# Unread products between two halves of a layer, a column copy shared by two engines, an earlier weight load, and low parts moved from GpSimd to VectorE

## The chip, the cores and the metric

The kernel runs on one core of one Trainium2 chip. The metric is the device time of one execution, in microseconds. The core has TensorE (PE, matrix products), VectorE (DVE), ScalarE (ACT), GpSimd (POOL) and SyncE (SP, which here only issues DMAs). SBUF is the on-chip memory in which operands lie, PSUM the one into which PE writes.

## What is computed

```python
# attention with hash buckets: 16 heads of 768 x 64
mask = q_bucket[:, :, :, None] == k_bucket[:, :, None, :]
scores = np.where(mask, scale * np.matmul(q, k.transpose(0, 1, 3, 2)), -1e9)
attn = exp(scores - max) / sum
x = (attn @ v), rearranged to (1536, 512)
# first mixture: each token goes to one of 8 experts
logits = x @ w_gate; expert_idx = argmax(logits, axis=1)
for e in range(8):
    xe = x[expert_idx == e]
    out[mask] = gate_w[mask, None] * (np.maximum(xe @ w1[e], 0.0) @ w2[e])   # 512 -> 1024 -> 512
# last layer, all 1536 tokens: 512 -> 1536 -> 512
xn = x / rms * rms_g
return silu(xn @ w_gate) * (xn @ w_val) @ w_out
```

All inputs and the output are float32.

## The kernel before

A float32 operand is held as two bf16 parts: the high part is read in place (the upper two bytes of each word, `upper[...]`), the low part is the difference, written by one subtraction. A product of two float32 matrices is three bf16 products: high by high, high by low, low by high.

**Attention** (to about 233 us) runs head by head, `h` from 0 to 15. PE makes scores (`score_tile`, `score_t_block`), ACT exponentiates them (L1076), and POOL writes the low parts of the probabilities tile by tile (`low_part(h, t)`, L1653) for t = 0, 1, 2, 4, 5; DVE does t = 3 (L1386). PE weighs the values of head h - 1 during head h; its first such product waits for all low parts of that head (`plo_ready`, before L685). The last head's values are weighed after all scores, tile by tile (L769 to L781).

**The first low part.** Ring slot 0 holds the first expert's first matrix (512 x 1024; per partition 4 row blocks `j` of 1024 columns). The low part of its left half is written in four pieces of 128 x 512, one for each j (`first_split`, L1687, semaphore `first_parts`), by POOL between its tiles: j = 0 and 1 after `value_low(15)` of head 14, ahead of `low_part(14, 4)`; j = 2 between `low_part(14, 4)` and `low_part(14, 5)`; j = 3 in head 15 behind `low_part(15, 2)`.

**Routing** (233 to 257 us): DVE works out each token's expert and place in a sorted order (L1404 to L1494), writes `one_hot` rows with which PE gathers the columns of unit 0 (L810) into `window[0]`, and POOL scatters all 1536 rows in sorted order to DRAM (12 indirect DMAs, L1728). From there three transposing DMAs (L586, issued by SP) bring the sorted columns back as `xT`, 8 planes (4 high, 4 low) of 1536 columns, 512 columns for each DMA.

**The mixture** runs ten units: eight experts and two spare ones. For unit u, `hidden(u, f)` (f = 0 to 7; L845, L846, L847) makes the first layer and `outputs(u)` (c = 0 to 3; L865 to L867) the second. PE's order: hidden(0), outputs(0), hidden(1), hidden(2), outputs(1), hidden(3), outputs(2), and so on. Each weight matrix is an item k in a ring of four slots. `split_half(k, side)` on POOL (L1675) writes the low part of half an item (128 x 2048) and raises `w_split`; POOL does these one behind the other from the end of its scatter: (0, 1), (1, 0), (1, 1), (2, 0), (2, 1), ... `hidden(u, 4)` waits for the second half of its item, `hidden(u, 0)` for the first, `outputs` for its item's halves at c = 0 and c = 2. Item 0 is hidden(0), 1 outputs(0), 2 hidden(1), 3 hidden(2), 4 outputs(1).

After each `hidden(u, f)` ACT writes the high part of the activations (L1104) and DVE the low part (L1500, `h_lo`); `outputs(u)` waits for all eight. For units u >= 1 the columns must be copied out of `xT` at a start known only at run time into `window[u % 2]`: `stage(u, planes)` on ACT (L1038), as planes 0 to 6 in one copy and plane 7 in a second, the latter raising `staged`, for which `hidden(u, 0)` waits. For unit 1 it waits for the first two transposes (`columns_in[0]`, `[1]`). Behind it in ACT's order stand the outputs of unit 0 (`take_output_block(0)`), then the activations of unit 1; unit 2's columns are staged in three pieces between those. DVE's order is: activations of unit 0, outputs of unit 0 (L1509, low parts of y), activations of unit 1.

**SP's order** there: the three transposes, a wait for `table_ready`, two register loads of the spare experts' numbers, then the loads of items 4, 5, ... , each behind `slot_free(k)`, which waits until PE has done with item k - 4 (L498 is `load_output`, L493 `load_hidden`).

**The last layer** (from about 410 us) is bound by PE and is not touched.

Of the kernel before, what the change touches and what calls it, by code (L numbers as in the profile page):

```python
# [25 lines left out]
NH = BATCH * HEADS  # L26
# [28 lines left out]
START_AT = 5  # L55
SPLIT_AT = [2, 5]
OUT_AHEAD = 2

# [110 lines left out]
def build(nc, qk, v, proj, w_router, w1, w2, w_gate, w_val, w_out, rms_g, consts, out):  # L171
# [14 lines left out]
    with ctx:  # L186
# [231 lines left out]
        wo_loaded = sem("wo_loaded")  # L418
        wo_split = sem("wo_split")
        staged = [sem(f"staged_{x}") for x in ("even", "odd")]  # L420
        h_ready = sem("h_ready")
        h_hi = sem("h_hi")
        h_lo = sem("h_lo")
# [32 lines left out]
        def _(sp):  # L456
# [127 lines left out]
            for c in range(ROUNDS):  # L584
                tokens = slice(c * GROUP, (c + 1) * GROUP)
                sp.dma_start_transpose(xT_parts.rearrange("p a j c -> p (a j) c")[:, :, tokens], parts[tokens, 0:2 * DM])\  # L586
                    .then_inc(columns_in[c], 16)
            sp.wait_ge(table_ready, 1)
            spare = [sp.value_load(table[0:1, T_EXPERT + n:T_EXPERT + n + 1], min_val=0, max_val=E - 1)
                     for n in range(OVER)]  # L590
            for k in range(RING, 2 * BLOCKS):
                slot_free(k)
                for u in range(BLOCKS):
                    if u >= E and k in (item_of_hidden(u), item_of_output(u)):
                        load_over(u, k, spare[u - E])
                    elif k == item_of_hidden(u):
                        load_hidden(u, u)
                    elif k == item_of_output(u):
                        load_output(u, u)
# [15 lines left out]
        def _(pe):  # L615
# [208 lines left out]
            def hidden(u, f):  # L824
                k, m = item_of_hidden(u), KF * u + f
                if f == 0:
                    if u:
                        pe.wait_ge(staged[u % 2], (u + 1) // 2)
                    else:
                        pe.wait_ge(first_columns, 2 * KD)  # L830
                if u == 0 and f == 0:
                    pe.wait_ge(first_parts, KD)
                elif f % (KF // 2) == 0:
                    pe.wait_ge(w_split, 2 * k + f // (KF // 2))
                if m >= 4:

                    pe.wait_ge(h_lo, m - 3)
                width = widths[u if u < E else u + OVER]
                o = bank(m % 4).shape_from_register(width)
                for j in range(KD):  # L840
                    c = j * F + f * P
                    w_hi, w_lo = upper[k % RING][:, c:c + P, 1], low[k % RING][:, c:c + P]
                    x_hi, x_lo = (window[u % 2][:, a, j, :] for a in range(2))
                    xh, xl = x_hi.shape_from_register(width), x_lo.shape_from_register(width)
                    mm(o, w_hi, xh, start=(j == 0), stop=False)  # L845
                    mm(o, w_hi, xl, start=False, stop=False)  # L846
                    last = mm(o, w_lo, xh, start=False, stop=(j == KD - 1))  # L847
                last.then_inc(h_ready, 1)
# [18 lines left out]
                        last = mm(o, w_lo, hh, start=False, stop=(f == KF - 1))  # L867
                    last.then_inc(y_ready, 1)

            for f in range(KF):  # L870
                hidden(0, f)
            for u in range(EARLY_WIDTHS, E):
                take_width(u)
# [162 lines left out]
        def _(act):  # L1036
# [74 lines left out]
            def stage(u, planes):  # L1111

                lo, hi = planes.start, planes.stop
                if lo == 0:
                    for c in range(2 if u == 1 else ROUNDS):
                        act.wait_ge(columns_in[c], 16)
                    if u > 1:
                        act.wait_ge(h_ready, KF * (u - 1))
                rows = xT[:, bass.ds(starts[u], 2 * KD * NTOK - NTOK + WMAX)]
                part = 2 * KD - 1  # L1120
                to = window[u % 2][:, :, :, :].rearrange("p a j c -> p (a j) c")
                last = copy(to[:, lo:min(hi, part), :],
                            rows[:, lo * NTOK:min(hi, part) * NTOK].rearrange("p (m c) -> p m c", c=NTOK)[:, :, 0:WMAX])
                if hi > part:
                    last = copy(to[:, part, :], rows[:, part * NTOK:part * NTOK + WMAX])
                    last.then_inc(staged[u % 2], 1)
# [19 lines left out]
                    act.wait_ge(table_ready, 1)  # L1146
                    take_start(1)
            act.wait_ge(scattered, 16 * TT)
            stage(1, slice(0, 2 * KD))
            take_output_block(0)  # L1150
            take_start(2)
            for f in range(KF):
# [101 lines left out]
        def _(dve):  # L1254
# [86 lines left out]
            def normalize(h):  # L1341
# [7 lines left out]
                if h >= 2:  # L1349
# [3 lines left out]
                V.tensor_tensor(x_head[h % 2][:, :, :], o[:, :, 0:D], scale.broadcast_to([P, T, D]), ALU.mult)\  # L1353
                    .then_inc(u_free, 1)

            def sum_logits(b):

                own.link(V.reduce_sum(L[:, b * T:(b + 1) * T, :].rearrange("p t e -> p (t e)"),
                                      logit_parts[:, b * T:(b + 1) * T, :, :].rearrange("p t e h -> p (t e) h"), AX.X))
# [12 lines left out]
            for h in range(NH):  # L1372
                if h >= 2:
                    normalize(h - 2)
                if h + 1 < NH:
                    for t in range(T):
                        reduce_tile(h + 1, t)
                        if t == 1 and h % 2 == 0 and h // 2 + 1 < PAIRS:
                            take_blend(h // 2 + 1)
                    maxima(h + 1)  # L1380
                if h == HEADS + 1:
                    dve.wait_ge(u_free, HEADS)
                    sum_logits(0)
                value_sum_rows(h)
                dve.wait_ge(exp_done, UNITS * h + 2 * DVE_TILE + 2)
                V.tensor_tensor(probs_lo[h % 2][:, DVE_TILE, :], probs[h % 2][:, DVE_TILE, :],  # L1386
                                probs_up[h % 2][:, DVE_TILE, :], ALU.subtract).then_inc(plo_dve_ready, 1)
                p = h // 2 + 2
                if h == hash_slot(p) and p < PAIRS:
                    signs(p)  # L1390
                    vt_low(p)
                if h and h % 2 == 0 and h // 2 + 1 < PAIRS:
                    query_low(h // 2 + 1)
# [3 lines left out]
            V.memset(psum[:, U_BANK:T_BANK + 1, 0:HALF], 0.0)  # L1397
            own.link(V.reduce_sum(L[:, T:TT, :].rearrange("p t e -> p (t e)"),
                                  logit_parts[:, T:TT, :, 0:HEADS - 1].rearrange("p t e h -> p (t e) h"), AX.X))

            last = bank(S_BANK)
            last_o, last_den = last[:, 0:T * UW].rearrange("p (t c) -> p t c", c=UW), last[:, DEN_COL:DEN_COL + T]
# [109 lines left out]
            dve.wait_ge(table_ready, 1)  # L1512
            for f in range(KF):
                take_hidden(0, f)
            take_output_block(0)
            for f in range(KF):
                take_hidden(1, f)
# [104 lines left out]
        def _(pool):  # L1622
# [68 lines left out]
            for h in range(NH):  # L1691
                for t in range(DVE_TILE):
                    low_part(h, t)
                if h == NH - 1:
                    first_split(KD - 1)
                if h == 0:
                    key_low(1)
                if h + 1 < NH:
                    value_low(h + 1)
                if h == NH - 2:  # L1700
                    first_split(0)
                    first_split(1)
                for t in range(DVE_TILE + 1, T):
                    low_part(h, t)
                    if h == NH - 2 and t == DVE_TILE + 1:
                        first_split(2)
                if h >= 2:
                    row_low(h - 2)
                if h == hash_slot(h // 2 + 2) and h // 2 + 2 < PAIRS:
# [104 lines left out]
```

## Time and profile before

| | us |
|---|---|
| median of 3 runs | 703.94 |
| the runs | 701.3, 703.94, 706.5 |
| the profiled execution | 704.02 |
| its span, first to last instruction | 702.2 |
| PE busy | 649.6 |
| POOL busy | 456.6 |
| DVE busy | 408.5 |
| ACT busy | 335.1 |

The profiled execution lies in the middle of the three runs; 1.8 us of it are outside the span. Times in the trace are microseconds from the start of the span. In a timeline a line gives start, duration, engine, line of the kernel, operation, output <- input, shape, and in brackets the idle time just before it with what ended it. Instructions of one engine overlap a little, so durations of neighbours can add up to more than the distance of their starts. "SPq" is SP's DMA queue, "PEclk" the granted clock of TensorE as a share of 2.4 GHz.

### The profile page before, as it was taken

Reading aid. Unit: us, or ns where it says so; the run is one execution under the profiler, and the core shown is the slowest. Engines: PE = TensorE matmul, PEld = TensorE weight load, DVE = VectorE, ACT = ScalarE, POOL = GpSimd, SP = SyncE. Lnnn points to the kernel's source line nnn. Section 1 sums busy time; section 2 is a strip of 40 time slices with the busy share of each in tenths; the row PEclk is TensorE's granted clock in tenths of the full one; section 3 lists DMA queues with packets and bytes.
Section 4 is the critical chain, followed back from the end, with each engine's and each line's share of the span. In section 5 each row is a group of like instructions: output and inputs, shape, how many; then the busy total and the mean of one; then the engine's idle time right before and its main releaser. Section 6 shows DMA issues by size and latency. Waiting matters only on the chain.

```text
span 702.2 us, 15710 instructions
## 1 busy us (share of the span) xinstructions
PE 649.6 (93%) x6576; PEld 448.1 (64%) x6588; DVE 408.5 (58%) x726; ACT 335.1 (48%) x581; POOL 456.6 (65%) x297
## 2 busy tenths in 40 slices
PE   3889999999999469999999989999999999999996
PEld 1256666766666469999999974444444444667773
DVE  6778888898884853544546743144344454544541
ACT  1355555555555235776667864242224233354332
POOL 5278768768779589898989974564437555451113
PEclk9999999999999789999999999999999999999999
DMA  6975765666488159876767990000001000010001
GB/s 174 245 175 128 174 170 127 167 159 146 92 242 343 40 186 230 327 281 243 273 244 283 335 380 24 1 1 1 1 0 61 0 1 1 1 60 2 1 1 60
DMA packets 59430, 94.43 MB, mean 134 GB/s; under 512 B 30208, under 2 KB 34432, under 8 KB 58336
## 3 DMA queue, kind: packets, MB, share of 16 engines
q1 hardware_dynamic: 57440, 87.12, 42.3%
q0 software_dynamic: 1920, 6.31, 2.4%
q8 instruction: 52, 0.85, 0.5%
q14 instruction: 18, 0.15, 0.1%
HBM read 76.98 MB, written 6.30 MB: 119 GB/s over the span
## 4 chain that ended last, share of the span: by engine, by line
PE 73%; DVE 12%; POOL 7%; DMA 3%; issue 2%; ACT 2%; SPq 1%; POOLq 0%; DVEq 0%; ACTq 0%
PE psum L920 6%; PE psum L921 6%; PE psum L919 6%; PE psum L986 4%; PE psum L987 4%; PE psum L988 4%; PE psum L651 3%; PE psum L865 3%; PE psum L866 3%; PE psum L867 3%; PE psum L845 3%; PE psum L846 3%; PE psum L847 3%; POOL low L1675 3%; PE psum L931 2%
## 5 line engine op out<-in xcount | busy, mean ns | idle before, releaser
L1653 POOL TENSOR_TENSOR probs_lo<-probs 128x768 bf16<-128x768 f32 x80 | 118.8, 1494 | 59.1 <-ACT probs L1076 58.9
L1675 POOL TENSOR_TENSOR low<-ring 128x2048 bf16<-128x2048 f32 x39 | 139.1, 3599 | 9.3 <-DMA ring<-in_moe_w 9.3
L1076 ACT ACTIVATE probs<-psum 128x384 f32<-128x384 f32 x192 | 92.4, 489 | 74.2 <-PE psum L666 71.5
L1777 POOL TENSOR_TENSOR s_lo<-gv,s_hi 128x512 bf16<-128x512 f32 x36 | 47.0, 1306 | 120.1 <-ACT s_hi L1038 120.0
L1319 DVE TENSOR_REDUCE psum<-psum 128x1 f32<-128x768 f32 x96 | 88.5, 960 | 16.3 <-PE psum L651 15.6
L865 PE MATMUL psum<-hT,ring 128*128 128x0 bf16 x320 | 68.7, 238 | 4.6 <-POOL low L1675 2.0
L921 PE MATMUL psum<-y,low 128*128 128x512 bf16 x192 | 72.9, 379 | 0.0
L920 PE MATMUL psum<-y,ring 128*128 128x512 bf16 x192 | 72.8, 379 | 0.0
L919 PE MATMUL psum<-y,ring 128*128 128x512 bf16 x192 | 72.8, 379 | 0.0
L867 PE MATMUL psum<-hT,low 128*128 128x0 bf16 x320 | 68.7, 238 | 0.0
L866 PE MATMUL psum<-hT,ring 128*128 128x0 bf16 x320 | 68.7, 238 | 0.0
L1500 DVE SCALAR_TENSOR_TENSOR hT<-psum,hT 128x512 bf16<-128x512 f32 x80 | 53.7, 689 | 25.2 <-ACT hT L1104 24.1
L685 PE MATMUL psum<-value,probs 128*128 128x73 bf16 x540 | 65.0, 200 | 2.4 <-POOL probs_lo L1653 1.4
L665 PE MATMUL psum<-head 128*128 128x384 bf16 x192 | 65.0, 339 | 0.8 <-ACT probs L1076 0.4
L686 PE MATMUL psum<-value_lo,probs 128*128 128x72 bf16 x540 | 65.0, 196 | 0.0
L687 PE MATMUL psum<-value,probs_lo 128*128 128x73 bf16 x540 | 65.0, 197 | 0.0
L666 PE MATMUL psum<-head 128*128 128x384 bf16 x192 | 64.2, 334 | 0.0
L1104 ACT ACTIVATE hT<-psum 128x512 bf16<-128x512 f32 x80 | 47.4, 598 | 30.3 <-PE psum L847 29.9
L651 PE MATMUL psum<-head 96*128 96x384 bf16 x192 | 51.0, 349 | 11.3 <-DVE psum L1319 9.0
L685 PEld LDWEIGHTS psum<-value,probs 128*128 128x128 bf16 x540 | 52.5, 97 | 9.7 <-POOL probs_lo L1653 1.8
L686 PEld LDWEIGHTS psum<-value_lo,probs 128*128 128x128 bf16 x540 | 53.2, 99 | 6.5
L986 PE MATMUL psum<-wo,s_hi 128*128 128x512 bf16 x144 | 55.8, 388 | 0.9 <-POOL s_lo L1777 0.5
(248 smaller groups left out, 1751.2 us busy)
## 6 DMA issues: line engine op xcount, KB each, us to landing
ring<-in_moe_w SPq DMA_DIRECT2D x20, 2048.0 KB, 9.0
pair_in<-in_qk SPq DMA_DIRECT2D x8, 1152.0 KB, 5.4
head<-in_qk SPq DMA_DIRECT2D x16, 384.0 KB
head<-in_qk SPq DMA_DIRECT2D x32, 192.0 KB, 5.2
head<-pair_in SPq DMA_DIRECT2D x32, 192.0 KB, 3.6
value<-in_v SPq DMA_DIRECT2D x16, 192.0 KB, 5.7
ring<-in_moe_w_gate SPq DMA_DIRECT2D x4, 768.0 KB, 10.1
ring<-in_moe_w_val SPq DMA_DIRECT2D x4, 768.0 KB, 11.1
```

The lines of the kernel that those rows point to most:

```text
L685: mm(o, p_hi, value_up[b][:, kt, :], start=(kt == 0), stop=False)
L686: mm(o[:, 0:VW], p_hi, value_lo[b][:, kt, :], start=False, stop=False)
L865: mm(o, w_hi, hh, start=(f == 0), stop=False)
L866: mm(o, w_hi, hl, start=False, stop=False)
L867: last = mm(o, w_lo, hh, start=False, stop=(f == KF - 1))
L919: mm(o, w_up[g][:, a, j, cols], yh, start=(j == 0), stop=False)
L920: mm(o, w_up[g][:, a, j, cols], yl, start=False, stop=False)
L921: last = mm(o, w_low[g][:, a, j, cols], yh, start=False, stop=(j == KD - 1))
L1076: nc.scalar.activation(probs[h % 2][:, t, half * HALF:(half + 1) * HALF], bank(ST_BANK + n % 2)[:, 0:HALF], ACT.Exp, scale=SCALE).then_inc ...
L1319: V.reduce_max(row_max[:, t // 2, t % 2:t % 2 + 1], psum[:, first:first + 2, 0:HALF], AX.XY).then_inc(s_free, 1)
L1653: G.tensor_tensor(probs_lo[par][:, t, :], probs[par][:, t, :], probs_up[par][:, t, :], ALU.subtract)\
L1675: G.tensor_tensor(half_of(lower, k, side), half_of(whole, k, side), half_of(high, k, side), ALU.subtract)\
```

## The change

1. Between hidden(0, 3) and hidden(0, 4) PE makes 18 products of 512 columns into PSUM bank 4 that nobody reads (`FILL`; the weights are the identity, the moving operand the upper halves of ring slot 0).
2. Unit 1's columns: ACT stages only planes 0 to 3; DVE copies planes 4 to 6 in one instruction and plane 7 in a second, between the activations and the outputs of unit 0. hidden(1, 0) waits for both.
3. SP issues the load of item 4 (the fifth load) behind the transposes and ahead of the wait for `table_ready` and the two register loads.
4. Of the four pieces of the first low part, POOL keeps j = 0 (same place) and j = 1 (now between `low_part(14, 4)` and `low_part(14, 5)`); j = 2 goes to DVE between `normalize(13)` and `value_sum_rows(15)`, j = 3 to DVE behind the sum of the logits of the second batch (L1398), ahead of its wait for the last head.

```diff
+FILL = 18
...
+        first_low_staged = sem("first_low_staged")
...
+            slot_free(RING)
+            load_output(1, 1)
             sp.wait_ge(table_ready, 1)
             spare = [sp.value_load(table[0:1, T_EXPERT + n:T_EXPERT + n + 1], min_val=0, max_val=E - 1)
                      for n in range(OVER)]
-            for k in range(RING, 2 * BLOCKS):
+            for k in range(RING + 1, 2 * BLOCKS):
...
                     if u:
                         pe.wait_ge(staged[u % 2], (u + 1) // 2)
+                        if u == 1:
+                            pe.wait_ge(first_low_staged, 1)
...
-            for f in range(KF):
+            for f in range(KF // 2):
+                hidden(0, f)
+            for _ in range(FILL):
+                mm(bank(4), ident[:, :], upper[0][:, 0:WMAX, 1], start=True, stop=True)
+            for f in range(KF // 2, KF):
                 hidden(0, f)
...
-            stage(1, slice(0, 2 * KD))
+            stage(1, slice(0, KD))
...
+            def first_split(j):
+
+                if j == 2:
+                    dve.wait_ge(w_loaded[0], 16)
+                    dve.wait_ge(blend_ready, PAIRS)
...
+                cols = slice(j * F, j * F + F // 2)
+                V.tensor_tensor(low[0][:, cols], ring[0][:, cols], upper[0][:, cols, 1], ALU.subtract).then_inc(first_parts, 1)
...
+                if h == NH - 1:
+                    first_split(2)
                 value_sum_rows(h)
...
                                   logit_parts[:, T:TT, :, 0:HEADS - 1].rearrange("p t e h -> p (t e) h"), AX.X))
+            first_split(3)
...
             for f in range(KF):
                 take_hidden(0, f)
+            start = dve.value_load(table[0:1, T_START + 1:T_START + 2], min_val=0, max_val=NTOK)
+            for c in range(2):
+                dve.wait_ge(columns_in[c], 16)
+            rows, end = xT[:, bass.ds(start, 2 * KD * NTOK - NTOK + WMAX)], 2 * KD - 1
+            V.tensor_copy(window[1][:, 1, 0:KD - 1, :],
+                          rows[:, KD * NTOK:end * NTOK].rearrange("p (m c) -> p m c", c=NTOK)[:, :, 0:WMAX])
+            V.tensor_copy(window[1][:, 1, KD - 1, :], rows[:, end * NTOK:end * NTOK + WMAX]).then_inc(first_low_staged, 1)
             take_output_block(0)
...
-                if h == NH - 1:
-                    first_split(KD - 1)
...
                 if h == NH - 2:
                     first_split(0)
-                    first_split(1)
                 for t in range(DVE_TILE + 1, T):
                     low_part(h, t)
                     if h == NH - 2 and t == DVE_TILE + 1:
-                        first_split(2)
+                        first_split(1)
```

## Rows read from the trace of the kernel before

**Rows 1.** The page: the span, and the granted TensorE clock in 40 slices.

```profile
span 702.2 us, 15710 instructions
PEclk9999999999999789999999999999999999999999
```

**Rows 2.** The page: the chain that ended last, share of the span by engine.

```profile
PE 73%; DVE 12%; POOL 7%; DMA 3%; issue 2%; ACT 2%; SPq 1%; POOLq 0%; DVEq 0%; ACTq 0%
```

**Rows 3.** Waits of PE, 185 to 310 us: us in total, times, longest.

```profile
PE psum L845 <- POOL low L1675: 4.6, 1, 4.6
PE psum L685 <- POOL probs_lo L1653: 1.4, 1, 1.4
```

**Rows 4.** Stretches, PE: us, busy us (instructions), granted clock, DMA share, GB/s.

```profile
228.70:232.70 4.00, 4.00 (x115) 1.00 0.23 70
256.60:259.60 3.00, 0.20 (x3) 1.00 0.45 175
259.60:261.38 1.78, 0.00 (x0) 0.50 0.03 7
261.38:267.70 6.32, 6.32 (x48) 0.60 1.13 230
269.35:277.28 7.93, 7.93 (x96) 1.00 0.99 170
```

**Rows 5.** Timeline, PE, 512-column products: start, us, line, operands.

```profile
561.48 0.39 PE L986 MATMUL psum<-wo,s_hi 128*128 128x512 bf16 x1
561.71 0.39 PE L987 MATMUL psum<-wo,s_lo 128*128 128x512 bf16 x1
```

**Rows 6.** Timeline, POOL, 214 to 233 us.

```profile
214.93 2.75 POOL L1687 TENSOR_TENSOR low<-ring 128x512 bf16<-128x512 f32 x2
220.07 1.46 POOL L1653 TENSOR_TENSOR probs_lo<-probs 128x768 bf16<-128x768 f32 x1
231.21 1.80 POOL L1660 TENSOR_TENSOR rows_out<-x_head,rows_out 128x384 bf16<-128x384 f32 x2
```

**Rows 7.** One line's DVE instructions (ns min/median/max), and timeline, DVE, 215 to 233 us.

```profile
L1386 DVE TENSOR_TENSOR probs_lo<-probs x16: 957/959/1611, 36.2 to 226.9; 128x768 bf16<-128x768 f32 x16
...
215.52 1.26 DVE L1386 TENSOR_TENSOR probs_lo<-probs 128x768 bf16<-128x768 f32 x1
218.44 0.56 DVE L1353 TENSOR_TENSOR x_head<-psum,rden 128x384 f32<-128x384 f32 x1
232.92 0.17 DVE L1404 TENSOR_SCALAR psum<-psum 128x6 f32<-128x6 f32 x1 [1.49 <-PE psum L771]
```

**Rows 8.** Timeline, ACT: unit 1's columns copied out of xT.

```profile
272.35 3.71 ACT L1038 ACTIVATE odd_window<-xT 128x3584 bf16 x2 [3.78 <-DMA xT<-sorted_x]
```

**Rows 9.** Timeline, POOL: the low parts running at 272 us and those after the next wait.

```profile
271.95 3.59 POOL L1675 TENSOR_TENSOR low<-ring 128x2048 bf16<-128x2048 f32 x1
284.50 7.16 POOL L1675 TENSOR_TENSOR low<-ring 128x2048 bf16<-128x2048 f32 x2 [1.85 <-DMA ring<-in_moe_w]
```

**Rows 10.** Timeline, POOL and DVE, at 236 us and from 484 us.

```profile
236.28 0.92 POOL L1660 TENSOR_TENSOR rows_out<-x_head,rows_out 128x384 bf16<-128x384 f32 x1 [3.26 <-ACT rows_out L1095]
236.29 0.92 DVE L1437 TENSOR_SCALAR table<-count 1x8 int32<-1x8 f32 x1
...
484.70 1.13 DVE L1572 TENSOR_TENSOR mix<-mix 128x128 f32<-128x128 f32 x1
485.75 1.26 DVE L1573 TENSOR_TENSOR mix<-mix 128x256 f32<-128x256 f32 x1
485.64 1.08 POOL L1739 TENSOR_TENSOR wo_lo<-wo 128x512 bf16<-128x512 f32 x1
```

**Rows 11.** Timeline, SyncE's queue.

```profile
259.81 13.81 SPq L586 DMA_TRANSPOSE xT<-sorted_x  x3
275.32 0.40 SPq L498 DMA_DIRECT2D ring<-in_moe_w  x1
```

**Rows 12.** Waits of PE, 345 to 420 us.

```profile
PE psum L865 <- POOL low L1675: 2.0, 1, 2.0
```

More of the change, by code:

```diff
@@ L1123, in stage @@
                             rows[:, lo * NTOK:min(hi, part) * NTOK].rearrange("p (m c) -> p m c", c=NTOK)[:, :, 0:WMAX])
+                if u == 1:
+                    last.then_inc(staged[u % 2], 1)
                 if hi > part:
@@ L1354, in normalize @@
                     .then_inc(u_free, 1)
+            def first_split(j):
+                if j == 2:
+                    dve.wait_ge(w_loaded[0], 16)
+                    dve.wait_ge(blend_ready, PAIRS)
+                    for h in (NH - 2, NH - 1):
+                        dve.wait_ge(parts_in[h % BUFS], 64 * (h // BUFS + 1))
+                        dve.wait_ge(score_in[h % BUFS], 48 * (h // BUFS + 1))
+                cols = slice(j * F, j * F + F // 2)
+                V.tensor_tensor(low[0][:, cols], ring[0][:, cols], upper[0][:, cols, 1], ALU.subtract).then_inc(first_parts, 1)
             def sum_logits(b):
```

## The prediction

> **What bounds the kernel now.** I read the page first: in the chain that ended last PE has 73%, DVE 12%, POOL 7% [rows 2], so the kernel is PE's work plus the places where PE stands still or runs slowly. The clock line over 40 slices of 17.6 us is below 9 tenths in two [rows 1]: slice 14 is the routing, which the change leaves as it is, and slice 15 (246 to 263 us) is where it works. The waits view for that part names PE's stalls [rows 3]: 4.6 us before hidden(0, 4), for the second half of the low part of item 0, which POOL can begin only after its scatter, and 1.4 us before L685, for POOL's low parts of head 14. The stretches [rows 4] show what the 4.6 us stall brings with it. PE goes idle at about 256.6; the clock is still full to 259.6, then at half (1.2 GHz) although nothing runs. The 48 products of hidden(0, 4..7) begin at 261.38 and need 6.32 us at a granted clock of 0.60; the 96 products of outputs(0) need 7.93 us at full clock, so 48 need 3.97. The stall therefore costs 2.35 us beyond itself. From 277.28 PE is in hidden(1). Behind it, PE's only named wait on another engine up to 420 us is 2.0 us [rows 12], for POOL. POOL is there driven by weight loads, and these are issued when PE frees a slot, so an earlier PE brings earlier loads: I pass on any gain at 277 us whole. All figures below are times of the profiled execution (704.02 us, span 702.2 [rows 1]); it lies 0.1 us from the median 703.94, so differences carry over.
>
> **The 18 unread products.** Two products of 512 columns with a moving operand read from SBUF start 0.23 us apart [rows 5]; 18 take 4.1 us, from 256.6 to 260.7, which ends 0.6 to 0.7 us before hidden(0, 4) could start anyway (261.38, set by POOL). Nothing waits for them. With PE busy the clock has no reason to fall; hidden(0, 4..7) ends 2.35 us sooner, and so does everything up to outputs(0), which would end at 277.28 - 2.35 = 274.9. The lower bound of the benefit is 0 (the clock falls all the same).
>
> **The low pieces in attention.** POOL spends two thirds of a tile's 1.46 us on a piece, 1.0 us (the first two took 2.75 because one of them stood behind DVE) [rows 6]. POOL loses j = 2 and j = 3, and j = 1 moves behind `low_part(14, 4)`. How much of it reaches PE needs care. What PE waits for is the end of `low_part(14, 5)`, 220.07 + 1.46 = 221.5 [rows 6]. DVE's L1386 shows how DVE and POOL share SBUF: 0.96 us in most of 16 cases, 1.26 at 215.52 and 1.6 at most [rows 7]. At 215.52 POOL was in its first piece (until 215.93); DVE stood until then, ran, and POOL's second piece had to stand in turn. A DVE instruction with two SBUF inputs and a POOL one thus take turns whole. In the new order: piece 0 until 215.93, L1386 until 216.7, `low_part(14, 4)` until 218.1, piece 1 until 219.1. DVE is free after L1353 (218.44 + 0.56 = 219.0 [rows 7]) and asks with piece 2 just ahead of that end; it goes first, with 512 of L1386's 768 columns at 0.86 us held, 0.6 us, to 219.7; `low_part(14, 5)` then ends at 221.15. PE gains 0.35 us. If DVE asks after 219.1, it is 0.95. That piece 3 leaves POOL in head 15 gives nothing: POOL's last low part ends at 231.2 (L1660 starts there [rows 6]), and DVE's wait for the last value product ends at 232.92 [rows 7], at the end of some 115 products that PE runs from 228.7 without a gap [rows 4]; they don't wait for POOL. Piece 3 on DVE falls into DVE's 1.49 us idle time ahead of that row; even if it stands behind POOL's L1660 for one of its 0.9 us, it fits or is late by 0.1 to 0.2. I take 0.35, range 0.1 to 0.95.
>
> **The shared copy.** I keep the clock of the trace before and shift at the end. ACT starts to copy at 272.35, released by the second transpose, and is done 3.71 us later at 276.06 [rows 8]. Half of the planes take half, to 274.2. DVE is idle at that time (its outputs of unit 0 wait for ACT), and its register load lies in that idle time too. What its two copies cost depends on POOL, which runs low parts of 3.59 us back to back, one from 271.95 to 275.5 [rows 9]. A copy of 512 in one run has one source, and a one-source instruction can stand as well: L1437, 8 elements in one partition, took 0.92 us beside POOL's L1660 of 0.92 us which began 0.01 us before it [rows 10]. So plane 7 waits for 275.5, then takes about 0.3: 275.85. For planes 4 to 6 the trace has no row. Lower bound: unhindered, 0.5 to 1.6 us, hidden behind the wait of plane 7. Upper bound: it too waits until 275.5, runs to 276.1, and POOL's next low part, queued meanwhile, goes ahead of plane 7. At 484 us this is seen: L1572 with 128 elements took 1.13, POOL's L1739 began at 485.64, and L1573, asked for at 485.75, took 1.26, that is it stood for all of L1739's 1.08 [rows 10]. Here it would be 3.59 us more, staged at 280.0. I take the lower bound: its source is three rows of 512 that lie 1536 apart and its target one run of 1536, so that source and target do not fall into the same two halves, unlike every row that stood here; this is inference and gets no more than its chance below.
>
> The Trainium skill (SBUF — State Buffer, "Who interferes with whom") says the same of the lock: whichever of a two-port DVE instruction and a GpSimd one starts first holds the shared pair for the whole instruction; by that rule alone this change's split is doubtful. L1386 at 1.26 against 0.96 agrees. The skill (Advanced Engine Details and Errata, on VectorE's performance modes) wants the outer counts of source and target both even, or odd and equal, for a two-port mode; 3 against one run would fail it, and the time would be that of my sum; no row here shows it.
>
> So hidden(1, 0) starts at the latest of PE (274.9), ACT (274.2) and DVE (275.85): 275.9 instead of 277.28, a gain of 1.4 us. Of the 2.35 us of the clock 1.0 is lost to plane 7. With ACT alone it would have been 276.1: in this sum the shared copy gives 0.2 us.
>
> **The earlier load.** SP issues item 4 at 275.32 [rows 11], 1.7 us after the last transpose left its queue (259.81 + 13.81 = 273.6); now at 273.65. The register loads move behind it; item 5's load was free to go only at 277.5, when PE ended outputs(0), and they end before that. POOL stood 1.85 us for item 4 until 284.50 [rows 9]; now it does not. But PE reads item 4 only in outputs(1), after two layers of 8 us or more from 277.3, at about 294; its first half was ready at 288.1. Hidden, worth 0; without it POOL would fall back by what PE gains, still covered by 6 us. Its traffic meets the third transpose, whose columns ACT needs only after hidden(1, 1), 2 us behind 277.3; I put no cost on it.
>
> **Sum.** 0.35 + 1.4 = 1.75 us less: 704.02 - 1.75 = 702.3.
>
> **The rivals.**
>
> A, the forecast, 702.3; its own range with the bounds 0.1 and 0.95 of the pieces and 0.2 either way for plane 7 is 701.5 to 702.7. Chance 0.53.
>
> B, both DVE copies stand behind POOL. PE ends outputs(0) at 274.9 and stands until 280.0, 2.7 us later than before. That idle time is longer than the one in which the clock fell (down 3 us after PE stopped [rows 4]), so hidden(1) pays what hidden(0) paid, 2.35. 704.02 + 2.7 + 2.35 - 0.35 = 708.7. It decides once the first copy has to wait past 274.9. For it: every hindered row; against: the shape. The shared copy would then be the cause of a slower kernel. Chance 0.14.
>
> C, no copy stands (both done by 273.8): start at 274.9, gain 2.4 + 0.35, 701.3. For it: the 3.59 us low parts have not been seen against such a copy; against: L1437. Chance 0.12.
>
> D, the unread products don't keep the clock, or the gain is lost in them: hidden(0, 4..7) as slow as before, outputs(0) ends at 277.28, everything staged by then, only the 0.35 remains: 703.7. For it: the clock's rise after such products isn't in this trace; against: the clock stays full through all stretches where PE is busy. Chance 0.09.
>
> The rest, 0.12, is for costs not listed, on both sides, mostly between 700 and 706.
>
> **Range and chances.** The three runs before spread from 701.3 to 706.5, so a median may lie 1.5 us from its execution. From C less 1.5 to D plus 2.3: 699.8 to 706.0, which leaves out B and a small part of the rest, under 0.2. A change under 1% (7 us) is about what a measurement of this kernel can't tell from none. No case reaches 696.9; B with 1.5 us of spread and something unlisted could reach 711. Faster by over 1% 0.05, within 1% 0.89, slower by over 1% 0.06.
>
> **What the new profile would show.** The clock line at 9 in slice 15; 18 products between 256 and 261; hidden(0, 4..7) in 4.0 us. L685 waiting 1.0 rather than 1.4 us. DVE's first copy under 1.7 us and the second ending just behind a boundary of two L1675 (A), or the first ending there and the second one low part later, with PE idle 5 us and a new dip of the clock (B), or both short (C). PE's wait ahead of the first product on `odd_window` is 1.0, 5 or 0 us. POOL without its wait for item 4. The prediction is wrong if the gain at hidden(1, 0) isn't found at the end, which would mean that a load or POOL, not PE, sets the later units.

## The result, and the profile after

The changed kernel takes 727.2 us (median of 4 runs, 726.8 to 730.1), the kernel before, run beside it, 705.0: a ratio of 1.032, 95% interval 1.029 to 1.035. The prediction was 702.3 us. The profiled execution after took 727.4 us with a span of 725.4, against 704.02 and 702.2 [rows 1].

The waits of PE from 185 to 330 us in the changed kernel (us in total, times, longest), in which L851, L871 and L689 are the lines that were L845, L865 and L685:

```profile
PE psum L851 <- issue: 20.8, 1, 20.8
PE psum L851 <- POOL low L1708: 2.7, 1, 2.7
PE psum L871 <- DVE hT L1526: 1.4, 1, 1.4
PE psum L689 <- POOL probs_lo L1686: 0.8, 1, 0.8
PE psum L851 <- ACT even_window L1048: 0.7, 1, 0.7
```

The first row is the loss: PE stands 20.8 us ahead of hidden(1, 0), for a semaphore that the view doesn't put down to an instruction. The timelines of DVE and of POOL (start, us, line, operands, count; POOL's rows are groups without a gap) show for what:

```profile
270.91 0.95 DVE L1545 COPY odd_window<-xT 128x1536 bf16 x1 [2.83 <-DMA xT<-sorted_x]
271.78 25.02 DVE L1547 COPY odd_window<-xT 128x512 bf16 x1
296.72 2.47 DVE L1535 TENSOR_TENSOR y<-psum,y 128x512 bf16<-128x512 f32 x4
...
257.47 39.18 POOL L1708 TENSOR_TENSOR low<-ring 128x2048 bf16<-128x2048 f32 x11
317.08 3.60 POOL L1708 TENSOR_TENSOR low<-ring 128x2048 bf16<-128x2048 f32 x1 [20.43 <-DMA ring<-in_moe_w]
```

The copy of planes 4 to 6 took 0.95 us while POOL worked. The copy of plane 7, a third of its size, took 25.02: it was asked for while POOL's fifth low part ran, six more came after it, and it ended at 296.80, when POOL's run ended (257.47 + 39.18 = 296.65). DVE got in at none of the boundaries between them. POOL's pause of 1.85 us at 282.65 in the kernel before [rows 9] is gone, as the early load was to make it.

The stretches of PE (us, busy us, instructions, granted clock, DMA share, GB/s), to be read beside [rows 4]:

```profile
258.30:260.80 2.50, 0.18 (x1) 0.99 0.15 58
260.80:261.13 0.33, 0.00 (x0) 0.50 0.05 14
261.13:267.70 6.57, 5.59 (x48) 0.77 1.15 217
276.30:297.01 20.71, 0.00 (x0) 0.62 0.46 178
297.01:303.00 5.99, 5.99 (x43) 0.61 0.02 4
```

Outputs(0) ended at 276.2 and hidden(1) began at 297.01, 19.7 us later than before (277.28 [rows 4]); outputs(1) began 21.7 later, since PE came back at the half clock (1.2 GHz, granted 0.61 in the last row). From there the distance is constant up to the end of the expert units (PE reaches the next stage at 430.05 instead of 408.52 us), so the loss at hidden(1) is nearly all of the 23.2 us by which the span grew. The remaining 1.7 us come behind it, where PE stood 1.0 us for DVE at 429 us and the granted clock of the next 41.5 us was 0.94 instead of 0.98.

### The profile page after: what moved, and what is told of

The parts are those of the page before. It is cut to its first block, busy times and chain, and to the rows that moved or that the text cites. A ratio compares the mean times of both kernels' runs of the same rounds, so it can differ in the third digit from the quotient of the medians.

```text
span 725.4 us, 15724 instructions
## 1 busy us (share of the span) xinstructions
PE 652.9 (90%) x6564; PEld 451.3 (62%) x6606; DVE 434.8 (60%) x730; ACT 334.1 (46%) x580; POOL 457.6 (63%) x295
## 4 chain that ended last, share of the span: by engine, by line
PE 73%; DVE 12%; issue 5%; POOL 4%; DMA 3%; ACT 1%; SPq 1%; POOLq 0%; DVEq 0%; ACTq 0%
PE psum L930 6%; PE psum L931 6%; PE psum L929 6%; PE psum L997 4%; PE psum L998 4%; PE psum L996 4%; PE psum L655 3%; PE psum L851 3%; PE psum L852 3%; PE psum L853 3%; PE psum L871 3%; PE psum L872 3%; PE psum L873 3%; PE psum L941 2%; PE psum L939 2%
## 5 line engine op out<-in xcount | busy, mean ns | idle before, releaser
L930 PE MATMUL psum<-y,ring 128*128 128x512 bf16 x189 | 71.6, 379 | 0.3
L871 PE MATMUL psum<-hT,ring 128*128 128x0 bf16 x320 | 68.0, 236 | 3.8 <-POOL low L1708 2.0
L929 PE MATMUL psum<-y,ring 128*128 128x512 bf16 x187 | 70.8, 379 | 0.2
L689 PE MATMUL psum<-value,probs 128*128 128x73 bf16 x540 | 65.0, 199 | 1.4 <-POOL probs_lo L1686 0.8
L689 PEld LDWEIGHTS psum<-value,probs 128*128 128x128 bf16 x540 | 52.5, 97 | 8.9 <-POOL probs_lo L1686 1.2
L997 PE MATMUL psum<-wo,s_lo 128*128 128x512 bf16 x142 | 54.9, 387 | 1.4 <-ACT o_sb L1202 0.6
```

What stands on the lines that cost most here:

```text
L689: mm(o, p_hi, value_up[b][:, kt, :], start=(kt == 0), stop=False)
L871: mm(o, w_hi, hh, start=(f == 0), stop=False)
L929: mm(o, w_up[g][:, a, j, cols], yh, start=(j == 0), stop=False)
L930: mm(o, w_up[g][:, a, j, cols], yl, start=False, stop=False)
```

## The experiments

**The copy alone, and the copy on ACT alone.** e2 is the kernel before with the shared copy only. e1 is the changed kernel with all eight planes on ACT again:

```diff
-            stage(1, slice(0, KD))
+            stage(1, slice(0, 2 * KD))
...
-            V.tensor_copy(window[1][:, 1, 0:KD - 1, :],
-                          rows[:, KD * NTOK:end * NTOK].rearrange("p (m c) -> p m c", c=NTOK)[:, :, 0:WMAX])
-            V.tensor_copy(window[1][:, 1, KD - 1, :], rows[:, end * NTOK:end * NTOK + WMAX]).then_inc(first_low_staged, 1)
```

> The changed kernel with unit 1's columns staged by ACT alone again; everything else of the change stays. Theory S (DVE's copy of plane 7 is starved by POOL's queued low parts, and that is the whole loss): PE starts hidden(1, 0) as soon as ACT is done, no idle time of 20 us, the kernel is 1 to 3 us faster than before, about 702. Rival R (the loss comes from another edit, or the three other edits cost together what the copy only shows): it stays slower than before by several us.

> The kernel before with the shared copy alone. Theory S: DVE's second copy lasts until POOL has no low part queued any more. The fifth load is issued as late as before, so POOL runs out of work for its wait on item 4 at about 282.7 us of the trace before, and the copy ends there: PE starts hidden(1, 0) at about 283 instead of 277.3, plus some 2 us for the clock, so 7 to 9 us slower than before, about 712, and not 22. Rival R2 (a copy of this form simply takes 25 us, or waits for something other than POOL): about 22 us slower.

Measured: e1 699.9 us, ratio 0.9952 (0.9932 to 0.9972); e2 711.8 us, 1.0133 (1.0101 to 1.0165). The shared copy is the whole loss; all the rest together makes the kernel 0.5% faster. In e2 (timelines of DVE and POOL):

```profile
272.06 9.96 DVE L1526 COPY odd_window<-xT 128x512 bf16 x1
...
256.93 24.93 POOL L1687 TENSOR_TENSOR low<-ring 128x2048 bf16<-128x2048 f32 x7
282.67 14.27 POOL L1687 TENSOR_TENSOR low<-ring 128x2048 bf16<-128x2048 f32 x4 [0.80 <-DMA ring<-in_moe_w]
```

The copy ended at 282.0, in the 0.80 us in which POOL waited for item 4 (from 281.86). In both kernels DVE got in when POOL ran out of work, and in e2 that was 15 us sooner, because item 4 was loaded late.

**Taking the collision away.** e3 makes POOL wait for the copies ahead of the second half of item 2 (`pool.wait_ge(first_low_staged, 1)`); e4 leaves planes 4 to 6 to DVE and gives plane 7 to ACT.

> The changed kernel; POOL waits for DVE's second copy (first_low_staged) ahead of the second half of item 2, so that no low part is queued behind the one that runs. Theory S: DVE's copy of plane 7 ends at the end of the low part in front of it, a copy of 0.3 to 0.5 us, no stall of PE over 1 us, 1 to 3 us faster than before, about 701.5. Rival R2: the copy still takes 20 us or more, and POOL and PE both stand for it: 725 or more.

> The changed kernel; DVE copies planes 4 to 6 only (three rows of 512 into one run of 1536), ACT planes 0 to 3 and plane 7. Theory S with the shape: DVE's copy takes 0.95 us beside POOL's low parts, as in the changed kernel, ACT's two take 1.9 and 0.6; no stall, 1 to 3 us faster than before. Rival (only the order of the two copies made the second the victim; any copy of DVE's is starved when POOL is queued at its time): the copy of three rows takes up to 25 us in some runs, 720 or more.

Measured: e3 700.4 us, 0.9968 (0.995 to 0.9987), the two copies 0.95 and 0.28 us; e4 700.5 us, 0.9963 (0.9943 to 0.9983), DVE's copy 0.95 us beside a running low part. Neither shows a wait at hidden(1). In e3 POOL had stopped at 270.6, before plane 7 was asked for at 271.20, so there was nothing to wait for. Plane 7 behind POOL was thus all of it, and planes 4 to 6 neither disturbed POOL nor waited for it.

**Which copies can stand.** e5 gives DVE two planes (4 and 5) in one instruction and nothing else, ACT the other six; e6 writes plane 7 as the maximum of the plane with itself, an instruction with two sources and the same values.

> The changed kernel; DVE copies planes 4 and 5 only (two rows of 512 into one run of 1024), ACT planes 0 to 3, 6 and 7. Theory P (the shape decides: a source whose outer count is even, like the target's, is read in two streams and needs what POOL holds): DVE's copy is starved until POOL stops, 20 us or more, about 727. Rival (one run of source is what is starved; rows are not): the copy takes about 0.7 us and the kernel is as with planes 4 to 6, 700 to 701.

> The changed kernel; plane 7 is written by DVE as the maximum of the plane with itself, a two-source instruction of the kind that took turns with POOL in attention. Theory W (a two-source instruction needs only a read path of POOL's and gets it at the end of the running low part; a one-source copy in two streams needs read and write paths, which POOL's overlapping instructions never leave free together): it waits for one low part at most, 3.6 us, PE starts hidden(1, 0) 0 to 2 us late, 700 to 703. Rival Q (whatever DVE asks for, it is starved while POOL's next instruction is queued with its waits met): 25 us, about 727.

The timelines of DVE in e5 (first row) and in e6 (second):

```profile
272.80 25.72 DVE L1546 COPY odd_window<-xT 128x1024 bf16 x1 [2.92 <-DMA xT<-sorted_x]
```

```profile
271.74 24.97 DVE L1548 TENSOR_TENSOR odd_window<-xT 128x512 bf16 x1
```

Each kernel was executed twice, and no ratio was formed. The profiled executions took 729.7 and 725.3 us, the other ones 710.9 and 709.9, about the time of e2. That would fit a POOL that stopped earlier in them, but there is no trace of either, and it is not shown. Three rows into one run go through, two rows into one run stand, two sources stand. The Trainium skill (Advanced Engine Details and Errata, "VectorE Performance Modes") asks for outer counts of source and target that are both even, or odd and equal, for a mode with two ports; where there is only one run, its columns are the count. All three copies here behave by that rule: 0.95 us for 3 rows into a run of 1536, 25.7 us for 2 rows into a run of 1024, and 25.0 us for one run of 512 into another.

**Does the length or the form of POOL's instruction matter?** e12 cuts POOL's low parts of items 2 and 3 into pieces of one row (128x512, as the first low part in attention).

```diff
+                step = 1 if k in (2, 3) else rows
+                for j in range(0, rows, step):
+                    a, b, c = (x[:, j:j + step, :] for x in parts)
+                    last = G.tensor_tensor(a, b, c, ALU.subtract)
```

> The changed kernel with POOL's four low parts of items 2 and 3 in pieces of one row (128x512, about 1 us each) with no wait between them. If what starves VectorE's copy is that POOL always has its next instruction queued, the copy is held as before, POOL loses 0.1 us or so a piece, and the time is 727 to 730. If VectorE gets in at the boundary of short or one-dimensional instructions (as it did in attention behind parts of 1.0 to 1.5 us), the copy ends 1 to 2 us after it was asked for, hidden(1) starts at about 274 us, and the time is 700 to 702.

Measured: 722.2 us, 1.0225 (1.0203 to 1.0248); plane 7 stood from 278.33 for 13.19 us, to the end of POOL's 33.81 us run of 21 instructions from 257.56. Instructions of 1 us let DVE in no more than those of 3.6. The time came out under the expected 727 to 730 because plane 7 was asked for 6.6 us later than in the changed kernel: ACT had stood before hidden(0, 0) (the stop told of below, 5.8 us here).

e14 puts three instructions that nothing reads behind the three-plane copy, while ACT does plane 7 (in e15 beside POOL's short pieces as well):

```diff
+            V.tensor_tensor(mix[:, 0:2 * P], cst[:, 0:2 * P], cst[:, 0:2 * P], ALU.subtract)
+            half = mix[:, WMAX:2 * WMAX].bitcast(BF16)
+            V.tensor_tensor(half[:, 0:WMAX], xT[:, 0:WMAX], xT[:, 0:WMAX], ALU.subtract)
+            V.tensor_copy(half[:, WMAX:2 * WMAX], xT[:, 0:WMAX])
```

> The changed kernel with plane 7 copied by ACT, and behind VectorE's copy of planes 4 to 6 three instructions whose results nothing reads, all with fixed addresses: a four-byte subtraction with two sources (256 columns), a two-byte subtraction with two sources (512), a two-byte copy in one run (512). If four-byte instructions take turns with GpSimd (as L1386 and L1573 did) and two-byte ones don't, the first ends within 4 us and the second lasts until GpSimd stops, at about 296. If the source address taken from a register was what held the copy, all three end within 4 us each. If whatever stands there waits while GpSimd has its next instruction queued, the first lasts 24 us. TensorE needs none of it before outputs(0)'s low values go on, but VectorE's outputs of unit 0 come behind it, so the time is near 700 in the first two cases only if VectorE is free soon, and above 710 otherwise.

> As e14, and GpSimd's low parts of items 2 and 3 in pieces of one row (128x512, 1.0 us), the form beside which L1386 got in. If the form and length of GpSimd's instruction decides together with VectorE's data type, the four-byte subtraction ends within 2 us here and lasts 24 us in e14; if it ends within 4 us in both, the data type or the address decides alone; if it lasts over 12 us in both, neither does.

Timelines of DVE and of POOL in e14 (713.6 us):

```profile
271.83 10.66 DVE L1548 TENSOR_TENSOR mix<-cst 128x256 f32<-128x256 f32 x1
282.42 0.41 DVE L1550 TENSOR_TENSOR mix<-xT 128x512 bf16<-128x512 bf16 x1
282.75 3.68 DVE L1551 COPY mix<-xT 128x512 bf16<-128x512 bf16 x1
...
257.27 24.94 POOL L1712 TENSOR_TENSOR low<-ring 128x2048 bf16<-128x2048 f32 x7
282.56 14.46 POOL L1712 TENSOR_TENSOR low<-ring 128x2048 bf16<-128x2048 f32 x4 [0.34 <-DMA ring<-in_moe_w]
```

In e15 (726.3 us; e14 and e15 are one execution each) the four-byte instruction stood 26.83 us. So the four-byte type of L1386 doesn't help, nor a fixed address: those theories fell. But the third row held a surprise. That copy was asked for at 282.75, when POOL had just begun four low parts back to back, and it ended at 286.43, at the first boundary between them. The same engines with the same instructions took turns there. What differed: POOL had paused 0.34 us at 282.2, for item 4, and before that pause not once since its last indirect DMA.

**A pause behind the scatter.** e16 is the changed kernel with one wait more, on POOL's own result:

```diff
             split_half(0, 1)
+            pool.wait_ge(w_split, 1)
             for k in range(1, 2 * BLOCKS):
```

> The changed kernel with one wait more: behind the low part that follows its scatter GpSimd waits until that part is done (about 0.1 us, at 258 to 261, ten us before VectorE's copies), and the rest of its low parts follow back to back as before. If the run of instructions that began behind the scatter is what shuts VectorE out, and a pause ends that, VectorE's copy of plane 7 ends at the next boundary of two low parts, within 4 us, TensorE starts hidden(1) by 276 and the time is 699 to 702. If any run in which GpSimd's next instruction is queued shuts it out, the copy lasts until GpSimd stops, 25 us, and the time is 725 to 728.

Measured: 701.3 us (10 runs), ratio 0.9974 (0.9954 to 0.9993). The timelines of DVE and of POOL:

```profile
270.06 0.95 DVE L1545 COPY odd_window<-xT 128x1536 bf16 x1 [4.90 <-DMA xT<-sorted_x]
270.92 3.19 DVE L1547 COPY odd_window<-xT 128x512 bf16 x1
...
256.00 25.13 POOL L1708 TENSOR_TENSOR low<-ring 128x2048 bf16<-128x2048 f32 x7
282.11 42.76 POOL L1708 TENSOR_TENSOR low<-ring 128x2048 bf16<-128x2048 f32 x12 [0.97 <-DMA ring<-in_moe_w]
```

The pause is so short that the view still counts seven low parts as one group. The first two of them alone are:

```profile
256.00 3.61 POOL L1708 TENSOR_TENSOR low<-ring 128x2048 bf16<-128x2048 f32 x1
259.69 3.60 POOL L1708 TENSOR_TENSOR low<-ring 128x2048 bf16<-128x2048 f32 x1
```

The second began 0.08 us after the end of the first; in the changed kernel it began 0.05 us ahead of it (257.47 and 3.61, then 261.03). From there on POOL's low parts start 3.56 us apart as before. The pause is over 11 us before DVE asks, POOL is as busy as before, and yet plane 7 now waits for one low part only: 3.19 us instead of 25. It took 26 us off the kernel (727.2 to 701.3).

e17 and e18 test the scatter itself. Both add one indirect DMA of POOL's, of a constant into rows that nothing reads, between items 0 and 1. In e17 the pause of e16 stands ahead of it, in e18 the only pause stands behind the low part that follows it.

```diff
                 if k == 1:
+                    G.indirect_dma_start(unread, bass.IndirectOffsetOnAxis(ap=pos[:, 0:1], axis=0),
+                                         cst[:, 0:2 * P], None).then_inc(unread_out, 16)
```

> e16 with one more indirect DMA of GpSimd (the first tile of a constant, 128x256, to rows in memory that nothing reads) between its pause and item 1, four low parts ahead of VectorE's copy. If an indirect DMA makes the run of instructions that follows it shut VectorE out until GpSimd pauses, VectorE's copy of plane 7 is held again over several low parts until GpSimd stops (10 to 25 us) and the time is 708 to 728. If the pause alone decided, the copy ends within 4 us and the time is 700 to 703 (the DMA costs GpSimd 1.3 us, which nothing waits for).

> The same indirect DMA at the same place, and the only pause behind the low part that follows it (first half of item 1), two low parts ahead of VectorE's copy. By the scatter theory the pause ends what the DMA began: the copy ends within 4 us and the time is 700 to 703. If the additional DMA hinders VectorE in some other way, the copy is late here too.

Timelines of POOL and DVE in e17 (725.7 us):

```profile
260.40 0.98 POOL L1767 DMA_INDIRECT unread_rows<-cst,pos  x1 [0.28 <-POOL low L1710]
261.42 35.60 POOL L1710 TENSOR_TENSOR low<-ring 128x2048 bf16<-128x2048 f32 x10
...
272.03 25.14 DVE L1549 COPY odd_window<-xT 128x512 bf16 x1
```

and in e18 (700.3 us):

```profile
260.57 0.99 POOL L1766 DMA_INDIRECT unread_rows<-cst,pos  x1 [0.17 <-issue]
261.59 71.40 POOL L1710 TENSOR_TENSOR low<-ring 128x2048 bf16<-128x2048 f32 x20
...
272.22 0.37 DVE L1549 COPY odd_window<-xT 128x512 bf16 x1
```

One indirect DMA brought the 25 us back; the pause behind it took them away, though POOL's run in e18 is the longest of all (20 low parts, 71 us). In e18 a boundary lay 0.2 us behind DVE's request, hence 0.37 us. In e17 one lay 0.1 us behind it (a low part from 268.53, of 3.59 us), and DVE was let in neither there nor at the six boundaries after it. Each is one execution, but they differ by 25 us, each in the direction foretold.

e7 had earlier put such a pause behind each of POOL's low parts of items 1 to 5; it fits too, but can't tell one pause from many:

> The changed kernel with DVE's two copies; POOL waits, behind each low part of items 1 to 5, for the semaphore which that low part raises, so that the next one is not started before it is finished. Theory O (the starving comes from POOL's next instruction starting while the last still drains, 3.59 us long at a spacing of 3.56): the gap of 0.1 us lets DVE's copy in at the first boundary, at about 275.5 of the trace before, copy of 0.3 us, PE starts hidden(1, 0) 1 us late at most, about 701. Rival Q: an engine that asks again at once wins again, the copy is starved as before, 727.

Measured: 701.2 us, 0.997 (0.995 to 0.999), plane 7 in 3.51 us.

**The other edits.** e8 has the unread products alone, e9 the moved low pieces alone, e10 the early load alone, e11 and e19 (the same kernel) all but the early load.

> The kernel before with the 18 unread products alone. By my prediction's term: hidden(0, 4..7) in 4.0 instead of 6.3 us, outputs(0) ends at 274.9 and hidden(1, 0) is held by ACT's staging until 276.1, so 1.2 us faster. Rival (the clock falls all the same or the products delay the rest): 0 or slower.

> The kernel before with only the pieces of the first low part spread (pieces 2 and 3 on VectorE, piece 1 later on POOL). By the waits of the changed kernel TensorE's wait for low_part(14, 5) shrinks by 0.55 us and the value sums of the last head by little, so 0.5 to 1.2 us faster, against the prediction's 0.35 (0.1 to 0.95). If pieces on VectorE beside POOL cost as much as they save: no change.

> The kernel before with only item 4's load issued earlier. POOL's wait of 1.85 us for it goes, and it is ahead of TensorE there by 6 us or more: no change (within 0.3% of the kernel before), as the prediction costed it at nothing. If the earlier load gets in the way of the column transposes, hidden(1) starts later and the time grows by as much.

> The changed kernel without its early load: item 4 is loaded after the register loads again, as in the kernel before. If the early load is what kept POOL without a gap, POOL stops for item 4 at about 281 to 282 us, VectorE's copy of plane 7 ends there (about 10 us instead of 25), hidden(1) starts at about 282, and the time is 708 to 711. If the early load has no part in the loss, the copy is held as long as in the changed kernel and the time stays at 726 to 728.

> The changed kernel with item 4's load back at its old place, as e11, run again. If the early load is what took away GpSimd's pause, GpSimd stops for item 4 at about 281 to 283 us, VectorE's copy of plane 7 ends there after about 10 us, TensorE waits 6 to 8 us ahead of hidden(1), and the time is 708 to 712 (ratio about 1.01). If the early load has no part in it, the copy lasts 25 us and the time is 725 to 728.

Measured: e8 701.7 us, 0.9984 (0.996 to 1.0007); e9 705.1, 0.999 (0.9969 to 1.0012); e10 707.4, 1.001 (0.9985 to 1.0034); e11 709.7, 1.0055 (1.0033 to 1.0077); e19 710.1, 1.0061 (1.0044 to 1.0077). None of the first three can be told from no change.

In e8 the clock held through hidden(0, 4..7). Of its stretches:

```profile
260.82:266.37 5.55, 4.13 (x48) 1.00 1.21 214
```

e11 and e19 fell into the range that was forecast for them (708 to 711 and 708 to 712), for another reason than the one written down. ACT's timeline in e11:

```profile
247.75 0.60 ACT L1046 ACTIVATE even_window<-psum 128x512 bf16<-128x512 f32 x1 [1.20 <-PE psum L812]
256.25 1.58 ACT L1046 ACTIVATE even_window<-psum 128x512 bf16<-128x512 f32 x3 [7.91 <-remote]
```

ACT stood 7.9 us among its copies of unit 0's columns, so hidden(0, 0) began at 257.9 instead of about 251. POOL's low part of item 0 was done at 258.2 (254.61 + 3.62), long before PE had finished hidden(0, 3) at 264.4, and the 18 unread products, which fill a wait in the other executions, now delayed hidden(0, 4) by their full 4.1 us. Plane 7, asked for at 275.30, was not let in at the boundary at 276.0 but stood until POOL's pause for item 4 at 279.6. That was before outputs(0) ended at 282.0, so it cost nothing. The rows thus repeat what e2 showed, that with the late load DVE gets in at POOL's pause. The times of these two kernels say how dear the unread products can be, and nothing on what the early load costs; for that e2 against the changed kernel stands. The same stop of ACT, 5.8 to 7.9 us, is in the profiles of e9, e10, e12 and e19 and in none of the others. In these five profiles it ends 1.7 us after POOL's last indirect DMA. The kernel before took 706.1 and 706.3 us beside these five and 702.9 to 703.7 beside the others, so it probably has the stop there as well. What ACT waits for in it stays open.

## Why the prediction was wrong, step by step

**The step that failed** is the one under the shared copy: "plane 7 waits for 275.5, then takes about 0.3". It rests on "A DVE instruction with two SBUF inputs and a POOL one thus take turns whole", read from L1386 [rows 7], on L1437 for an instruction with one source, and, for the upper bound, on L1573 [rows 10]. Those rows are right: L1386 did get in between two of POOL's instructions. But each of them comes from a place where POOL had issued no indirect DMA yet (attention, and 236 us, ahead of the scatter) or had paused often since (484 us). Plane 7's copy met POOL in the one run of low parts that followed the scatter without a pause, a state of which the trace of before holds no collision. Rival B priced one low part more (708.7); the true price had no upper end but POOL's running out of work.

With the state taken away the step is right. In e16, which is the changed kernel plus one pause, plane 7 ended at 274.1 just behind a boundary of two low parts, PE waited 1.0 us for it, and the ratio was 0.9974 (0.9954 to 0.9993); the forecast was 702.3 / 704.02 = 0.9976. From hidden(0, 4) to hidden(1, 0) e16 takes 274.32 - 259.67 = 14.65 us against 277.28 - 261.38 = 15.9 before [rows 4], a gain of 1.2 where the sum had 1.4.

**The earlier load was costed at nothing, "hidden"**. Alone it shows no difference (e10). But the question asked of it was whether anyone waited for item 4, not whether anyone lived on POOL's waiting for it. The pause of 1.85 us [rows 9] would have let DVE in 10 us after its request (e2, 1.0133); with the load moved, POOL ran on to 296.65 (1.032). The loss was about 9 us in e2 and 22 us in the changed kernel, so more than half of it hangs on an edit that had no term in the sum. This is read from e2 against the changed kernel; the direct test, e11 and e19, was spoiled by ACT's stop.

**The unread products** were right in mechanism and size where they reached up to POOL's low part: hidden(0, 4) to outputs(0) took 5.55 us in e8, against 261.38 to 269.35, 7.97, before, so 2.4 us for the predicted 2.35. In the profiled execution after they didn't reach: they ended at 258.5, POOL's part only at 261.1, PE stood 2.65 us, the clock fell to the half at 260.8, and the same way took 7.0 us. The reason was POOL, whose first indirect DMA took 3.90 us there beside DVE's one_hot instead of 1.21 (see the last section). Of the 2.4 us, 1.1 arrived at hidden(1) in e8, which then waited 1.1 us, until ACT's copies were done (271.80 + 3.71 = 275.5): the prediction had 1.2 with ACT alone.

**The low pieces**: PE's wait for head 14 went from 1.4 [rows 3] to 0.8 us, in the changed kernel and in e9: 0.6 where the sum had 0.35, inside its 0.1 to 0.95. DVE asked just ahead of the end of POOL's piece and went before `low_part(14, 5)`, as supposed, and held it for 0.45 us (1.91 against 1.46) where the sum had 0.6.

**Planes 4 to 6** were right: 0.95 us, not hindered, in every kernel that has this copy. The shape, on which this was a guess, was the reason: two rows instead of three stood (e5). **What the shared copy is worth** was small, as said: without it (e1) hidden(1) waits 0.15 us for ACT. And a delay at hidden(1) does pass whole to the end, as said of a gain, with the half clock behind the long wait on top of it (19.7 us at hidden(1), 21.7 at outputs(1)).

**The range** left out B and anything beyond it. The chance of 0.14 for B was a chance that a copy stands once more; none was given to its standing without end, though the sum itself said that POOL runs its low parts back to back there, which was the reason to ask.

## What to carry to other kernels

Before giving DVE a copy in one run, or anything with two sources in SBUF, beside a queue of POOL work, look at what POOL did last: if it issued indirect DMAs and has not paused since, the instruction may stand until POOL does. Three things helped here: three rows into one run (e4), the copy on ACT (e1, e4), and one wait of POOL for its own result behind the scatter (e16, a pause of 0.08 us). When a wait is removed, ask who else was using it. And filler products for the clock are free only while the wait that they fill is there in every execution.

## What the hardware showed that was not expected

- A run of POOL instructions that followed an indirect DMA without a pause shut out DVE's copies of one row and of two, a two-byte instruction with two sources and a four-byte one, and let through only the copy of three rows: 25.0 us over seven low parts, 26.8 us over parts of 3.6 and 1.0 us (e15), against one part (3.2 us) after a pause of 0.08 us (e16). A pause for POOL's own result (e7, e16, e18) and one for a DMA (e14) both ended it. e17 and e18 tie it to the indirect DMA, with one execution each. What in the engine is held from the DMA to the pause isn't visible in a trace and stays open. The Trainium skill (SBUF — State Buffer, "Who interferes with whom") gives the shared pair to whoever issues first "for the whole instruction"; e16's 3.19 us agrees, the 25.02 us over seven instructions do not.
- The indirect DMAs themselves vary: the first beside DVE's run of one_hot took 1.2 us in the kernel before and in all others but two, 3.90 in the changed kernel and in e5. Timeline of POOL, changed kernel:

```profile
239.58 3.90 POOL L1758 DMA_INDIRECT sorted_x<-rows_out,pos  x1 [4.87 <-DVE pos L1483]
243.79 0.96 POOL L1758 DMA_INDIRECT sorted_x<-rows_out,pos  x1 [0.30 <-issue]
```

  DVE's one_hot ran from 238.53 for 4.84 us there, and the DMA ended at 243.48, 0.1 us behind the end of that run; in e5 it is 245.13 and 245.01. So in these two POOL stood for the whole of DVE's run, the other way round than with plane 7; why only in these two stays open. The twelve DMAs took 17.9 us instead of 15.6, which made POOL 2.2 us late at item 0, and that left the clock to fall there.
- ACT's stop of 5.8 to 7.9 us, released by "remote", told of above.
